# Attention over five start-up rounds: downsampled exponentials read straight from the scores' bank, and a new order of each engine's steps in a round

## The chip, the cores and the metric

The kernel runs on one core of one Trainium2 chip. The metric is the device time of one execution in microseconds (us); the kernel before took 924.17 us (median of three runs). All engines of the core run their own instruction streams and meet through semaphores: TensorE (PE; weight loads are shown apart as PEld), VectorE (DVE), ScalarE (ACT), GpSimd (POOL) and the queue SyncE (SP) that issues nearly all transfers.

## The reference, cut to what matters

For 4 batches of 8 heads, 576 positions and head size 64, attention is the sum of two branches, and its result goes through a gated layer and a squared-ReLU layer.

```
def sm_attn(qq, kk, vv):
    s = scale * np.matmul(qq, kk.transpose(0, 1, 3, 2))
    s = s - np.max(s, axis=-1, keepdims=True)
    a = np.exp(s)
    a = a / (np.sum(a, axis=-1, keepdims=True) + 1e-09)
    return np.matmul(a, vv)
q_d, k_d, v_d = ...          # means over groups of 4 positions: 144 positions
out_up = np.repeat(sm_attn(q_d, k_d, v_d), 4, axis=2)
mask = np.abs(pos[:, None] - pos[None, :]) < 4
...                          # out_local: softmax attention inside the mask
attn = out_up + out_local
x = silu(x @ w_gate) * (x @ w_val) @ w_out     # 2304 tokens, 512 -> 1536 -> 512
h = np.maximum(x @ w_in, 0.0)                  # 512 -> 2048 -> 512
return h * h @ w_out
```

## The kernel before, in words

Heads are taken in pairs: 4 pairs make a batch (`PAIRS`), 16 pairs make the whole input. Pairs 0 to 3 are computed in five **rounds** (n = 0 to 4) with little else to do for TensorE. From then on there are 48 **slots** in which the dense products of the first weight pass of one batch fill TensorE while the attention of the next pairs is spread between them, and then the chunks of the two layers with a seven-product scheme. The rounds occupy the first 47 us; the change is in them alone.

Each round n works on three pairs at once. What happens to one pair i, by names and lines:

- `pe_scores_loc` (L757) writes banded scores into the banks `sc`: two mask products (L763) and 40 small ones (L774). `dve_maximum_loc` (L1483) takes maxima (L1490) and writes scores minus maximum to `probs_l` (L1494), which frees `sc` for the next pair. `act_exp_loc` (L1166) takes exponentials in place; `dve_normalise_loc` (L1498) sums, adds, inverts, multiplies (L1503 to L1509), with its small sums kept in the last columns of bank `sd`. `pe_turn_loc1` and `pe_turn_loc2` transpose the result (L793, tile `tr`), ACT copies it out (L1178, L1182).
- `pe_scores_ds` (L779) writes the downsampled scores, three tiles of 144 columns, into bank `sd` (L788). `dve_maximum_ds` (L1512) takes maxima (L1515) and writes scores minus maximum to `probs_d` (L1519). `act_exp_ds` (L1169) takes exponentials of `probs_d` in place, one instruction of 432 columns (L1171). `dve_normalise_ds` (L1523) sums (L1527), adds, inverts, multiplies (L1534). `pe_turn_ds` transposes in two halves, each copied out by ACT (`act_move_ds`, L1189).
- `pe_values_loc` (L866) and `pe_values_ds` (L848) multiply by the values. ACT copies the downsampled part (`act_move_ods`, L1197), `dve_sum_branches` (L1545) adds the branches, `act_split_x` (L1206) and POOL's `split_x_lo` (L642) split the sum into a rounded part and a rest for the dense products.
- `pe_keep_busy` (L875) issues products whose result nobody reads: 8 in round 0 after the first scores, then 4, 4 and 5 in a middle round, 2 in the last.

**Feeding.** POOL makes the sums of four positions: `downsample_qk` (L613 to L623, for the next pair) and `downsample_v` (L631 to L636). The tile `v_grp` that the latter reads has one buffer: SP issues the load for the next pair (L384) only when `downsample_v` is done (`s_vds`), and everything behind it in SP's queue (weights L424, q and k L358, value windows L368 and L374) waits with it. POOL runs in its written order: in round 1 `downsample_qk(2)`, the rest of weight unit 0 (`first_weight_lo`, L675), `downsample_v(1)`; in round 2 `downsample_qk(3)`, `split_x_lo(0)`, `downsample_v(2)`; in round 3 `downsample_qk(4)`, `split_x_lo(1)`, `downsample_v(3)`, weight unit 1; then `split_x_lo(2)`. `first_weight_lo(i)` needs ACT's rounded copy of the weights (`act_weight`, L1275), which ACT makes for unit 0 in round 1, unit 1 in round 2 and unit 2 in round 3 (`ROUND_HI`), ahead of the first copy of transposed probabilities.

`pe_scores_ds(n)` opens round n on PE, ahead of `pe_scores_loc(n + 1)`. The first slot's dense product over pair 2 waits for the first half of `split_x_lo(2)` (`s_xlo`).

Of the kernel before, what the change touches and what calls it, by code (L numbers as in the profile page):

```python
# [165 lines left out]
def mlp_kernel(nc, qT, kT, v, w1_in, w1_out, w2_in, w2_out, out):  # L166
    ctx = ExitStack()
    with ctx:
        def sb(name, shape, dt=F32):
            return ctx.enter_context(nc.sbuf_tensor(name, shape, dt))  # L170
# [39 lines left out]
        ident = sb("ident", [P, P])  # L210
        max_l = sb("max_l", [P, 2, TJ])
        max_d = sb("max_d", [P, DT])
        credits = sb("credits", [P, 2])

        def late(name, shape, offset, dt=F32):
# [492 lines left out]
        def _(g):  # L708
# [26 lines left out]
            for ps in range(1, PASSES):  # L735
# [3 lines left out]
                for m in range(MT):  # L739
                    pool_out_lo(g, ps, m)  # L740

        def sums_loc(k):


            return sd[:, DT * DS + 2 * TJ * k:DT * DS + 2 * TJ * (k + 1)]
# [32 lines left out]

        def pe_scores_ds(pe, i):  # L779
            if i > 0:  # L780
                pe.wait_ge(s_subd, i)
                pe.wait_ge(s_norml, i)
            if i > PAIRS:
                pe.wait_ge(s_normd, i)
            pe.wait_ge(s_qkds, 3 * i + 3)
            for q in range(DT):
                for h in range(2):
                    last = nc.tensor.matmul(sd[64 * h:64 * h + 64, DS * q:DS * (q + 1)],  # L788
                                            q_ds[:, h, DQ * q:DQ * q + 64], k_ds[:, :], start=True, stop=True)
            last.then_inc(s_sd, 1)  # L790
# [81 lines left out]
        def pe_keep_busy(n):  # L872

            for _ in range(n):
                nc.tensor.matmul(mlp_ps[0][:, 0:LOC], ident16[:, :],  # L875
                                 mask[:, 0:TJ, :].rearrange("p j k -> p (j k)"), start=True, stop=True)

        def pe_round(pe, n):
            if n == 0:
                pe_scores_loc(pe, 0)  # L880
                pe_keep_busy(8)
            pe_scores_ds(pe, n)
            if n < PAIRS:
                pe_scores_loc(pe, n + 1)
            if n == PAIRS:
                pe_keep_busy(2)
                pe_first_in(pe, 0, 0, 0, 0, 0, KT - 2)
            if n > 0:
                pe_turn_ds(pe, n - 1, 0)
                if n < PAIRS:  # L890
                    pe_keep_busy(4)
                pe_turn_ds(pe, n - 1, 1)
                pe_values_loc(pe, n - 1)
                pe_values_ds(pe, n - 1)
            if n < PAIRS:
                pe_keep_busy(4)
                pe_turn_loc1(pe, n)
                pe_keep_busy(5)
                pe_turn_loc2(pe, n)

        def pe_slot(pe, g):
# [266 lines left out]

        def act_exp_ds(a, i):  # L1169
            a.wait_ge(s_subd, i + 1)  # L1170
            nc.scalar.activation(probs_d[:, :], probs_d[:, :], ACT.Exp, scale=SCALE / FACTOR ** 2)\  # L1171
              .then_inc(s_expd, 1)

        def act_move_loc1(a, i):
            a.wait_ge(s_turn1, i + 1)
# [33 lines left out]

        def act_round(a, n):  # L1210
            last = n == PAIRS
            if not last:
                act_exp_loc(a, n)
            for i in ROUND_HI.get(n, []):
                act_weight(a, i)
            if n > 0:
                act_move_ds(a, n - 1, 0)
            if n > 1:
                act_split_x(a, n - 2)
            if n > 0:  # L1220
                act_move_ds(a, n - 1, 1)
                if last:
                    act_exp_loc(a, n)
                act_move_ods(a, n - 1)
            if last:
                act_split_x(a, n - 1)
                act_exp_ds(a, n)
                return
            act_move_loc1(a, n)
            act_exp_ds(a, n)  # L1230
            act_move_loc2(a, n)

        def act_slot(a, g):

# [277 lines left out]
        def dve_maximum_ds(d, i):  # L1512
# [10 lines left out]
        def dve_normalise_ds(d, i):  # L1523
            total, den, inv = (sums_ds(i, k) for k in range(3))
            pd = probs_d[:, :].rearrange("p (q k) -> p q k", q=DT)
            d.wait_ge(s_expd, i + 1)
            nc.vector.tensor_reduce(total, pd, AX.X, ALU.add).then_inc(s_sumd, 1)  # L1527
            d.wait_ge(s_sumd, i + 1)
# [21 lines left out]

        def dve_round(d, n):
            last = n == PAIRS
            if not last:
                dve_maximum_loc(d, n)
            if n > 0:
                dve_normalise_ds(d, n - 1)
            if n > 1:
                dve_sum_branches(d, n - 2)
            if last:
                dve_maximum_loc(d, n)  # L1560
            if last:
                dve_sum_branches(d, n - 1)
                dve_maximum_ds(d, n)
                dve_normalise_loc(d, n)
            else:
                dve_normalise_loc(d, n)
                dve_maximum_ds(d, n)

        def dve_slot(d, g):
            for i in pairs_in(7, g):  # L1570
# [310 lines left out]
```

## Time and profile before

| | |
|---|---|
| median of 3 runs | 924.17 us (920.74 to 924.63) |
| the profiled execution | 926.48 us |
| its span in the trace | 924.7 us |
| outside the span | 1.8 us |
| TensorE busy | 909.2 us (98%) |
| VectorE, ScalarE, GpSimd busy | 650.9, 400.4, 219.8 us |
| granted TensorE clock, mean | 0.996 |

A row of the timeline has the start in us, the duration, the engine, the line and operation, the tile written and the tiles read with their shapes, how many instructions were merged, and in brackets the idle time of the engine ahead of it with what ended it. A tile name in a row is that of the program without buffer numbers; `mlp_ps` and `sd` are banks of PSUM. The profiled execution is 2.3 us longer than the median run.

### The profile page before, as it was taken

To read this page: it belongs to the slowest core of one execution; us is meant where nothing else is said; L and a number is where in the kernel's file an instruction comes from. 1 tells how busy PE (TensorE), PEld (TensorE's weight loads), DVE (VectorE), ACT (ScalarE), POOL (GpSimd) and SP (SyncE) were. 2 spreads that over 40 slices of the span, in tenths; PEclk is the share of its full clock that TensorE was granted. 3 is DMA by queue.
4 is the path that set the end of the run, shared out by engine and by line. 5 is a ranking of instruction groups with operands and counts; after the bars stand their busy time and mean duration, and the time that the engine had idled before them with its cause. 6 is when DMAs were issued, how large, how long until landed. Compare 5 with 4: busy or idle time off the path is not lost.

```text
span 924.7 us, 17274 instructions
## 1 busy us (share of the span) xinstructions
PE 909.2 (98%) x6762; PEld 879.0 (95%) x6762; DVE 650.9 (70%) x1112; ACT 400.4 (43%) x733; POOL 219.8 (24%) x278
## 2 busy tenths in 40 slices
PE   8899999999999999999999999999999999999998
PEld 5698999999999999999999999999999999999998
DVE  7685756564576757796757799585879575778775
ACT  3474555554446343455343445242535242525331
POOL 5784545452262000422000223000313000202000
PEclk9899999999999999999999999999999999999999
DMA  9953333231242020421311230010332020221422
GB/s 219 220 175 105 105 103 97 72 99 32 87 126 68 2 69 1 123 83 35 103 35 69 74 133 1 1 35 1 103 103 69 0 70 1 80 80 35 137 69 69
DMA packets 70881, 71.38 MB, mean 77 GB/s; under 512 B 27280, under 2 KB 58000, under 8 KB 70800
## 3 DMA queue, kind: packets, MB, share of 16 engines
q1 hardware_dynamic: 68496, 65.55, 24.3%
q10 hardware_dynamic: 2304, 4.72, 1.5%
q8 instruction: 54, 0.88, 0.4%
q14 instruction: 27, 0.22, 0.1%
HBM read 56.10 MB, written 14.16 MB: 76 GB/s over the span
## 4 chain that ended last, share of the span: by engine, by line
PE 85%; DVE 6%; ACT 3%; DMA 2%; issue 2%; POOL 1%; SPq 1%; ACTq 0%; DVEq 0%; POOLq 0%
PE mlp_ps L975 13%; PE mlp_ps L977 12%; PE mlp_ps L976 12%; PE sc L975 5%; PE sc L977 5%; PE sc L976 5%; PE xp L977 4%; PE xp L975 4%; PE xp L976 4%; PE sd L975 3%; PE sd L977 2%; PE sd L976 2%; PE tr L975 2%; PE tr L977 2%; PE tr L976 2%
## 5 line engine op out<-in xcount | busy, mean ns | idle before, releaser
L1388 ACT ACTIVATE wh_hi<-hbuf 128x384 fp32r<-128x384 f32 x144 | 70.8, 522 | 79.5 <-DVE hbuf L1674 57.1
L694 POOL TENSOR_TENSOR w_raw<-w_raw 128x256 f32<-128x256 f32 x16 | 14.3, 894 | 355.4 <-DMA w_raw<-w_in 355.4
L1682 DVE TENSOR_TENSOR wh_lo<-hbuf,wh_hi 128x384 fp32r<-128x384 f32 x144 | 76.5, 560 | 24.5 <-ACT wh_hi L1388 21.0
L1637 DVE TENSOR_TENSOR ring<-ring_raw,ring 128x768 fp32r<-128x768 f32 x96 | 90.9, 969 | 0.0
L1337 ACT ACTIVATE ring<-ring_raw 128x768 fp32r<-128x768 f32 x96 | 75.3, 836 | 28.8 <-DVE ring_raw L1631 28.5
L975 PE MATMUL mlp_ps<-ring,w_hi 128*128 128x384 f32 x240 | 80.3, 334 | 0.4 <-ACT snap L1368 0.4
L977 PE MATMUL mlp_ps<-ring,w_lo 128*128 128x384 f32 x240 | 80.2, 334 | 0.0
L976 PE MATMUL mlp_ps<-ring,w_hi 128*128 128x384 f32 x240 | 80.2, 334 | 0.0
L975 PE MATMUL mlp_ps<-wh_hi,w_hi 128*128 128x384 f32 x216 | 73.0, 338 | 2.3 <-DVE wh_lo L1682 1.2
L976 PE MATMUL mlp_ps<-wh_lo,w_hi 128*128 128x384 f32 x216 | 72.2, 334 | 0.0
L977 PE MATMUL mlp_ps<-wh_hi,w_lo 128*128 128x384 f32 x216 | 72.2, 334 | 0.0
L977 PE MATMUL sc<-wh_hi,w_lo 128*128 128x384 f32 x216 | 72.2, 334 | 0.0
L976 PE MATMUL sc<-wh_lo,w_hi 128*128 128x384 f32 x216 | 72.2, 334 | 0.0
L975 PE MATMUL sc<-wh_hi,w_hi 128*128 128x384 f32 x216 | 72.1, 334 | 0.0
L975 PE MATMUL mlp_ps<-xin,w_hi 128*128 128x288 f32 x216 | 65.9, 305 | 0.0
L976 PE MATMUL mlp_ps<-xin,w_hi 128*128 128x288 f32 x216 | 63.7, 295 | 0.0
L977 PE MATMUL mlp_ps<-xin,w_lo 128*128 128x288 f32 x216 | 63.5, 294 | 0.0
L704 POOL TENSOR_TENSOR w_lo<-w_raw,w_hi 128x512 fp32r<-128x512 f32 (+1 forms) x20 | 30.5, 1545 | 138.6 <-ACT w_hi L1311 138.6
L1674 DVE SCALAR_TENSOR_TENSOR hbuf<-hbuf 128x384 f32<-128x384 f32 x96 | 57.2, 629 | 1.4
L1362 ACT ACTIVATE hbuf<-sd 128x384 f32<-128x384 f32 x24 | 11.8, 492 | 99.3 <-PE sd L977 99.3
L975 PE MATMUL sd<-ring,w_hi 128*128 128x384 f32 x144 | 48.3, 335 | 0.6 <-ACT snap L1368 0.4
L976 PE MATMUL sd<-ring,w_hi 128*128 128x384 f32 x144 | 48.1, 334 | 0.0
(208 smaller groups left out, 2671.7 us busy)
## 6 DMA issues: line engine op xcount, KB each, us to landing
ring_raw<-x_whole SPq DMA_DIRECT2D x24, 384.0 KB, 3.7
ring_raw<-y_whole SPq DMA_DIRECT2D x24, 384.0 KB, 3.7
qk_sb<-qT SPq DMA_DIRECT2D x16, 288.0 KB, 3.3
qk_sb<-kT SPq DMA_DIRECT2D x16, 288.0 KB, 4.2
v_grp<-v SPq DMA_DIRECT2D x32, 144.0 KB
x_whole<-x_f ACTq DMA_DIRECT2D x16, 288.0 KB, 2.3
y_whole<-ypart SPq DMA_DIRECT2D x3, 1536.0 KB, 6.3
v_win<-v SPq DMA_DIRECT2D x64, 64.0 KB, 2.8
```

Of the source, the lines that this page charges most:

```text
L694: nc.gpsimd.tensor_tensor(block(5), block(7), block(4), ALU.add).then_inc(s_usum[i], 1)
L704: nc.gpsimd.tensor_tensor(w_lo[:, a:a + n], w_raw[:, a:a + n], w_hi[:, a:a + n].bitcast(F32), ALU.subtract).then_inc(s_olo[m], 1)
L975: nc.tensor.matmul(o, wh, xh, start=first, stop=False, skip_group_check=more)
L976: nc.tensor.matmul(o, wh, xl, start=False, stop=False, skip_group_check=more)
L977: return nc.tensor.matmul(o, wl, xh, start=False, stop=last, skip_group_check=more)
L1337: nc.scalar.activation(ring[:, SLOTS[g][p], 0, :, :], whole(g, p), ACT.Copy).then_inc(s_ophi, 1)
L1362: nc.scalar.activation(made_in(g, n, 0), BANK_1[n % 2], ACT.Copy).then_inc(s_snap1, 1)
L1388: nc.scalar.activation(hi[:, f, t, :], hbuf[:, e, :], ACT.Copy).then_inc(s_shhi, 1)
L1637: nc.vector.tensor_tensor(ring[:, SLOTS[g][p], 1, :, :], whole(g, p), ring[:, SLOTS[g][p], 0, :, :].bitcast(F32), ALU.subtract).then_inc(s ...
L1674: nc.vector.scalar_tensor_tensor(hbuf[:, e, :], hbuf[:, e, :], 0.0, hbuf[:, e, :], ALU.max, ALU.mult).then_inc(s_m, 1)
L1682: nc.vector.tensor_tensor(lo[:, f, t, :], hbuf[:, e, :], hi[:, f, t, :].bitcast(F32), ALU.subtract)\
```

## The change

For pairs 0 to 3 the subtraction of the maximum (L1519) and the separate row sum (L1527) go away. VectorE only scales the three maxima into a shift (`shift_d`), and ScalarE reads the scores from bank `sd` itself, in three instructions of 144 columns, each with its shift as bias and its row sum as second output (`total_d`). So bank `sd` stays taken until ScalarE is through: `pe_scores_ds` and `dve_normalise_loc`, whose sums lie in the same bank, wait for it. Round 4's pair (4) keeps the old form.

The order of each engine in a round is changed with it. PE: `pe_scores_ds(n + 1)` is issued at the end of round n between the two transposes of the local probabilities; `pe_scores_loc(n + 1)` stands between the two halves of `pe_turn_ds(n - 1)`; keep-busy products are 2 and 2 in a middle round. ACT: `act_move_ds(n - 1, 0)` leads, both exponentials follow, and `act_weight` goes to the very end of the round. VectorE: `dve_normalise_ds(n - 1)` leads, `dve_maximum_loc`, `dve_maximum_ds`, `dve_sum_branches(n - 2)` and `dve_normalise_loc` follow. POOL's and SP's own orders are untouched.

```diff
         def pe_scores_ds(pe, i):
             if i > 0:
-                pe.wait_ge(s_subd, i)
+                if i <= PAIRS:
+                    pe.wait_ge(s_expd, exps_ds(i))
+                else:
+                    pe.wait_ge(s_subd, i)
                 pe.wait_ge(s_norml, i)
...
         def pe_round(pe, n):
+            last = n == PAIRS
             if n == 0:
                 pe_scores_loc(pe, 0)
                 pe_keep_busy(8)
-            pe_scores_ds(pe, n)
-            if n < PAIRS:
-                pe_scores_loc(pe, n + 1)
-            if n == PAIRS:
+                pe_scores_ds(pe, 0)
+            if n > 0:
                 pe_keep_busy(2)
+            if last:
                 pe_first_in(pe, 0, 0, 0, 0, 0, KT - 2)
             if n > 0:
                 pe_turn_ds(pe, n - 1, 0)
-                if n < PAIRS:
-                    pe_keep_busy(4)
+            if not last:
+                pe_scores_loc(pe, n + 1)
+            if n > 0:
                 pe_turn_ds(pe, n - 1, 1)
                 pe_values_loc(pe, n - 1)
                 pe_values_ds(pe, n - 1)
-            if n < PAIRS:
-                pe_keep_busy(4)
+            if not last:
+                pe_keep_busy(2)
                 pe_turn_loc1(pe, n)
-                pe_keep_busy(5)
+                pe_scores_ds(pe, n + 1)
                 pe_turn_loc2(pe, n)
...
         def act_exp_ds(a, i):
             a.wait_ge(s_subd, i + 1)
-            nc.scalar.activation(probs_d[:, :], probs_d[:, :], ACT.Exp, scale=SCALE / FACTOR ** 2)\
-              .then_inc(s_expd, 1)
...
+            if i > 0:
+                a.wait_ge(s_turnd, 2 * i)
+                a.wait_ge(s_dend, i)
+            for q in range(DT):
+                cols = slice(DS * q, DS * (q + 1))
+                nc.scalar.activation(probs_d[:, cols], sd[:, cols], ACT.Exp, bias=shift_d[:, q:q + 1],
+                                     scale=SCALE / FACTOR ** 2, accum_out=total_d[:, q:q + 1]).then_inc(s_expd, 1)
...
         def act_round(a, n):
             last = n == PAIRS
+            if n > 0:
+                act_move_ds(a, n - 1, 0)
             if not last:
                 act_exp_loc(a, n)
-            for i in ROUND_HI.get(n, []):
-                act_weight(a, i)
+                act_exp_ds(a, n)
             if n > 0:
-                act_move_ds(a, n - 1, 0)
+                act_move_ds(a, n - 1, 1)
             if n > 1:
                 act_split_x(a, n - 2)
...
             act_move_loc1(a, n)
-            act_exp_ds(a, n)
             act_move_loc2(a, n)
+            for i in ROUND_HI.get(n, []):
+                act_weight(a, i)
...
         def dve_normalise_loc(d, i):
             d.wait_ge(s_expl, i + 1)
             d.wait_ge(s_sd, i + 1)
+            if i < PAIRS:
+
+                d.wait_ge(s_expd, exps_ds(i + 1))
...
         def dve_maximum_ds(d, i):
-            if i > 0:
-                d.wait_ge(s_turnd, 2 * i)
+            if i < PAIRS:
+                if i > 0:
+                    d.wait_ge(s_expd, exps_ds(i))
+                nc.vector.tensor_scalar(shift_d[:, :], max_d[:, :], -SCALE / FACTOR ** 2, 0.0, ALU.mult, ALU.add)\
+                  .then_inc(s_subd, 1)
+                return
...
         def dve_normalise_ds(d, i):
+            d.wait_ge(s_expd, exps_ds(i + 1))
+            if i < PAIRS:
+                total = total_d[:, :]
+            else:
+                nc.vector.tensor_reduce(total, pd, AX.X, ALU.add).then_inc(s_sumd, 1)
```

`exps_ds(n)` counts the exponentials of the first n pairs: three for each of pairs 0 to 3, one from pair 4 on.

## Rows read from the trace of the kernel before

**Rows 1.** The page: busy time by engine, and the transfers' share in 40 slices.
```profile
PE 909.2 (98%) x6762; PEld 879.0 (95%) x6762; DVE 650.9 (70%) x1112; ACT 400.4 (43%) x733; POOL 219.8 (24%) x278
...
DMA  9953333231242020421311230010332020221422
```

**Rows 2.** Busy time of each engine in the stretch behind the rounds.
```profile
43.46:100.00 56.54, 55.91 (x700) 50.82 (x699) 41.70 (x80) 33.52 (x66) 37.28 (x51) 1.00 0.47 135
```

**Rows 3.** The chain that ended last, 0 to 64 us: start, us, what.
```profile
25.89 8.51 DMA ypart<-w_in
...
46.78 0.64 PE xp L848 x8
```

**Rows 4.** Timeline of ACT in the rounds.
```profile
13.13 0.55 ACT L1171 ACTIVATE probs_d<-probs_d 128x432 f32<-128x432 f32 x1
...
16.14 1.06 ACT L1275 ACTIVATE w_hi<-ypart 128x1024 fp32r<-128x1024 f32 x1 [0.73 <-DMA ypart<-w_in]
...
25.57 0.39 ACT L1189 ACTIVATE probsT_d<-tr 72x288 f32<-72x288 f32 x1
...
28.01 0.29 ACT L1197 ACTIVATE o_ds<-xp 128x144 f32<-128x144 f32 x1 [1.03 <-PE xp L848]
...
34.43 1.06 ACT L1275 ACTIVATE w_hi<-ypart 128x1024 fp32r<-128x1024 f32 x1 [3.47 <-DMA ypart<-w_in]
```

**Rows 5.** Timeline of PE in the rounds.
```profile
8.67 0.96 PE L788 MATMUL sd<-k_ds,q_ds 128*64 128x144 f32 x12
...
22.74 1.34 PE L774 MATMUL sc<-qk_sb 64*58 64x64 f32 x40
...
26.02 0.52 PE L793 MATMUL tr<-ident,probs_d 128*72 128x128 f32 x3 [0.94 <-ACT probsT_d L1189]
...
35.83 0.85 PE L793 MATMUL tr<-ident,probs_d 128*72 128x128 f32 x3 [2.29 <-ACT probsT_d L1189]
```

**Rows 6.** Two 1 us stretches; last: granted clock, DMA share, GB/s.
```profile
35.00:36.00 1.00, 0.17 (x1) 0.17 (x2) 0.11 (x1) 1.00 (x3) 0.99 (x2) 0.82 0.86 203
...
42.00:43.00 1.00, 1.00 (x11) 0.66 (x11) 0.70 (x2) 0.51 (x2) 0.86 (x2) 0.77 0.79 128
```

**Rows 7.** Timeline of DVE, rounds 2 and 3.
```profile
23.98 0.82 DVE L1503 TENSOR_REDUCE sd<-probs_l 128x10 f32<-128x640 f32 x1
...
25.30 0.82 DVE L1509 TENSOR_TENSOR probs_l<-probs_l,sd 128x640 f32<-128x640 f32 x1
...
26.68 0.61 DVE L1519 TENSOR_TENSOR probs_d<-sd,max_d 128x432 f32<-128x432 f32 x1
...
28.05 0.82 DVE L1494 TENSOR_TENSOR probs_l<-sc,max_l 128x640 f32<-128x640 f32 x1
...
30.12 0.61 DVE L1527 TENSOR_REDUCE mlp_ps<-probs_d 128x3 f32<-128x432 f32 x1 [1.25 <-ACT probs_d L1171]
30.77 0.17 DVE L1530 TENSOR_SCALAR mlp_ps<-mlp_ps 128x3 f32<-128x3 f32 x1
...
32.45 0.82 DVE L1503 TENSOR_REDUCE sd<-probs_l 128x10 f32<-128x640 f32 x1
```

**Rows 8.** Timeline of POOL in the rounds.
```profile
22.75 0.73 POOL L631 TENSOR_TENSOR v_tmp<-v_grp 72x256 f32<-72x256 f32 x1 [3.11 <-DMA v_grp<-v]
...
27.53 0.48 POOL L623 TENSOR_TENSOR k_ds<-qk_tmp 128x144 f32<-128x144 f32 x1
...
40.84 0.72 POOL L631 TENSOR_TENSOR v_tmp<-v_grp 72x256 f32<-72x256 f32 x1 [1.72 <-DMA v_grp<-v]
...
43.08 2.36 POOL L675 TENSOR_TENSOR w_lo<-ypart,w_hi 128x1024 fp32r<-128x1024 f32 x1
45.88 1.55 POOL L642 TENSOR_TENSOR xin<-x_f,xin 128x288 fp32r<-128x288 f32 x2 [0.44 <-ACT xin L1206]
```

**Rows 9.** Timeline of the queue SP: issues of the `v_grp` loads.
```profile
25.05 0.79 SPq L384 DMA_DIRECT2D v_grp<-v  x2
...
34.69 0.77 SPq L384 DMA_DIRECT2D v_grp<-v  x2
```

More of the change, by code:

```diff
@@ L212, in mlp_kernel @@
         max_d = sb("max_d", [P, DT])
+        shift_d = sb("shift_d", [P, DT])
+        total_d = sb("total_d", [P, DT])
         credits = sb("credits", [P, 2])
@@ L740, in _, with exps_ds @@
                     pool_out_lo(g, ps, m)
+        def exps_ds(n):
+            return DT * min(n, PAIRS) + max(n - PAIRS, 0)
         def sums_loc(k):
@@ L1170, in act_exp_ds @@
             a.wait_ge(s_subd, i + 1)
-            nc.scalar.activation(probs_d[:, :], probs_d[:, :], ACT.Exp, scale=SCALE / FACTOR ** 2)\
-              .then_inc(s_expd, 1)
+            if i >= PAIRS:
+                nc.scalar.activation(probs_d[:, :], probs_d[:, :], ACT.Exp, scale=SCALE / FACTOR ** 2)\
+                  .then_inc(s_expd, 1)
+                return
[6 more added lines that the diff above has]
+                                     scale=SCALE / FACTOR ** 2, accum_out=total_d[:, q:q + 1]).then_inc(s_expd, 1)
         def act_move_loc1(a, i):
@@ L1211, in act_round @@
             last = n == PAIRS
+            if n > 0:
+                act_move_ds(a, n - 1, 0)
             if not last:
                 act_exp_loc(a, n)
-            for i in ROUND_HI.get(n, []):
-                act_weight(a, i)
+                act_exp_ds(a, n)
             if n > 0:
-                act_move_ds(a, n - 1, 0)
+                act_move_ds(a, n - 1, 1)
             if n > 1:
                 act_split_x(a, n - 2)
+            if last:
+                act_exp_loc(a, n)
             if n > 0:
-                act_move_ds(a, n - 1, 1)
-                if last:
-                    act_exp_loc(a, n)
                 act_move_ods(a, n - 1)
@@ L1516, in dve_maximum_ds @@
             d.wait_ge(s_maxd, i + 1)
-            if i > 0:
-                d.wait_ge(s_turnd, 2 * i)
+            if i < PAIRS:
[3 more added lines that the diff above has]
+                  .then_inc(s_subd, 1)
+                return
+            d.wait_ge(s_turnd, 2 * i)
             nc.vector.tensor_tensor(probs_d[:, :].rearrange("p (q k) -> p q k", q=DT), tiles,
@@ L1525, in dve_normalise_ds @@
             pd = probs_d[:, :].rearrange("p (q k) -> p q k", q=DT)
-            d.wait_ge(s_expd, i + 1)
-            nc.vector.tensor_reduce(total, pd, AX.X, ALU.add).then_inc(s_sumd, 1)
-            d.wait_ge(s_sumd, i + 1)
+            d.wait_ge(s_expd, exps_ds(i + 1))
[3 more added lines that the diff above has]
+                nc.vector.tensor_reduce(total, pd, AX.X, ALU.add).then_inc(s_sumd, 1)
+                d.wait_ge(s_sumd, i - PAIRS + 1)
             nc.vector.tensor_scalar(den, total, EPS, float(FACTOR), ALU.add, ALU.mult).then_inc(s_dend, 1)
@@ L1552, in dve_round @@
             last = n == PAIRS
-            if not last:
-                dve_maximum_loc(d, n)
             if n > 0:
                 dve_normalise_ds(d, n - 1)
-            if n > 1:
+            if last:
                 dve_sum_branches(d, n - 2)
-            if last:
                 dve_maximum_loc(d, n)
-            if last:
                 dve_sum_branches(d, n - 1)
                 dve_maximum_ds(d, n)
-                dve_normalise_loc(d, n)
             else:
-                dve_normalise_loc(d, n)
+                dve_maximum_loc(d, n)
                 dve_maximum_ds(d, n)
+                if n > 1:
+                    dve_sum_branches(d, n - 2)
+            dve_normalise_loc(d, n)
         def dve_slot(d, g):
```

## The prediction

> **What bounds the kernel now.** I read the page first: TensorE is busy 98% of the span [rows 1]. Then the busy time by stretch: behind the rounds it is busy 55.91 of 56.54 us [rows 2], so from about 47 us on the work is rigid, and the change can only move the moment at which that dense work begins. The chain of waits for the first 64 us came third. It shows that the rounds are not bound by one engine. A weight load of 8.51 us sits in the chain, and the last step of the rounds, the downsampled values of pair 3, starts at 46.78 and ends at 47.42 [rows 3]. That 47.42 is the mark I move below; the dense product over pair 2 follows it directly.
>
> The timelines say why. On ScalarE the rounded copy of weight unit 2 waits 3.47 us for its load, and everything behind it on ScalarE waits too [rows 4]. TensorE then stands 2.29 us before the second half of a transpose, where the round before had 0.94 [rows 5], and in this gap the granted clock falls: 0.82 on average in the microsecond from 35, 0.77 in that from 42, with 0.5 between, so slow from about 35.64 to 42.46 [rows 6]. Those are 6.8 us at 1.2 instead of 2.4 GHz; the same transposes took 0.85 us instead of 0.52 [rows 5]. At that ratio of 1.63 the slow stretch cost 6.8 x (1 - 1/1.63) = 2.6 us. Beside this a second chain runs, through transfers and POOL: the value load for `downsample_v` is what POOL waits for, 3.11 us before 22.75 and 1.72 us before 40.84 [rows 8], and the transfer engines are at nine tenths or more in the first two slices of 23 us each [rows 1].
>
> **The change on VectorE and ScalarE.** VectorE loses the subtraction (0.61) and the sum (0.61) and gains a shift like the 0.17 us scaling: 1.05 us a round less [rows 7]. A round of VectorE ran 32.45 - 23.98 = 8.47 us, 1.25 of it idle before the sum [rows 7]; its own work was thus 7.2 and becomes about 6.2. ScalarE loses one exponential of 0.55 us and gains three of 144 columns. The nearest row, a copy of 128x144 out of PSUM, is 0.29 [rows 4]. No row shows an accumulator output or a bias per partition. From below the three cost no less than the one they replace, 0.55; from above I let each need a second instruction of the same 0.29, 1.74 in all. I take 1.1, near three times 0.29 with a little for the sums.
>
> The Trainium skill, page "ScalarE: Activation LUTs", section "What ACT_TABLE_LOAD costs", gives 280 ns + 0.833 ns a column for an exponential with a pointer bias and an overlap of 93 ns. An estimate by that page is three times 0.40 less two overlaps, 1.0 us, without a price for the sum. That speaks against splitting one instruction into three; the sum of this text does not use it.
>
> **One middle round, new order.** I count from N, the end of the local normalisation on VectorE. TensorE: first transposes and downsampled scores, about 0.6 and 0.9; copy and last transpose and copy, to N + 2.0; fillers and first transpose half, to 2.6. VectorE meanwhile has finished `dve_normalise_ds` (sum gone, 0.95) and `dve_maximum_loc` (twice 0.82 [rows 7]), at 2.6 too. Local scores of the next pair, 0.3 + 1.34 [rows 5], to 4.3; second transpose half (0.52), to 4.8. Only then may ScalarE write `probs_d`: exponentials to 5.9. Only then may VectorE touch the bank: local normalisation, from the row 23.98 to the end of the row 25.30 2.14 us [rows 7], to 8.1. So the new round is 8.1 us long. The added wait costs what it hides: behind the waiting normalisation nothing is queued on VectorE but the next round, and TensorE waits for it after its last two fillers. VectorE's 1.05 us is gone into that wait: the round is bound by a chain TensorE - ScalarE - VectorE, not by VectorE. Against the undisturbed round of 8.47 this is 0.4 shorter, against its busy part longer.
>
> **Start.** Round 0: the downsampled scores are in at 8.67 + 0.96 = 9.63 [rows 5], maximum 0.6, shift 0.2, exponentials 1.1, normalisation 2.15 and some 0.2 of signals: N0 = 13.9 (before, that normalisation went ahead of the downsampled maxima). N1 = 22.0, N2 = 30.1 by the period.
>
> **The moved weight copies.** `act_weight` now stands last. What goes: ScalarE's 3.47 us stall, with the 1.35 us it added to TensorE's gap and the 2.6 of the slow clock. What comes: unit 0 is copied at N1 + 2.0 = 24.0 to 25.1 instead of 16.14 [rows 4]. POOL's rest of unit 0 (2.37 [rows 8]) then runs to 27.5, `downsample_v(1)` (43.08 - 40.84 = 2.25 [rows 8]) to 29.7, `downsample_qk(3)` (28.01 - 22.75 - 2.25 = 3.0 [rows 8]) to 32.7. Before, the latter ended at 27.53 + 0.48 = 28.0; 3.1 of the 7.9 us were covered by POOL's wait, the rest is not. TensorE wants these sums for the scores of pair 3 at N2 + 0.6 = 30.7: 2.0 late, the only delay of the main chain. N3 = 30.1 + 8.1 + 2.0 = 40.2. The copies of units 1 and 2 wait for nothing by then: unit 2's load landed at 34.4 [rows 3], also when issued 4 us later it is there at 42.
>
> From N3: transposes, scores of pair 4, last transpose 1.8, fillers and the first dense products 1.1, two transpose halves with their copies (0.5 and 0.39 each [rows 4, 5]) 1.8: TensorE could do the values of pair 3 at 44.9 and be done at 45.6, 1.8 before the mark.
>
> **The other chain.** POOL on: `split_x_lo(0)` 1.55 [rows 8] to 34.2, `downsample_v(2)` to 36.5, `downsample_qk(4)` to 39.5 (TensorE wants it at 40.8, fine), `split_x_lo(1)` to 41.0, then `downsample_v(3)`. Its load landed at 40.84 before, issued at 34.69 [rows 8, 9]. Now it is issued behind `downsample_v(2)` and SP's other issues, about 36.8. SP is also held from 25.05 [rows 9] to 29.7 by the load before that one. I take the landing as unchanged, since the transfer engines have work queued for that long: a load issued at 25.89 landed 8.5 us later [rows 3]. So `downsample_v(3)` ends at 43.3, unit 1 (2.36 [rows 8]) at 45.7, the first half of `split_x_lo(2)` at 46.5. Before, it ended at 45.88 + 0.8 = 46.7 and was covered by TensorE's values to 47.42. Now it is what TensorE's first product over pair 2 waits for. The mark moves from 47.42 to 46.5: a gain of 0.9 us. The main chain's other 0.9 is lost behind POOL. So dropping 3.47 us of stall and 2.6 us of slow clock brings one: the value load, POOL's fixed order and the later weight unit take the rest.
>
> **Sum.** 926.48 - 0.9 = 925.6 us for a profiled execution; the median stands 2.3 lower, 924.17 - 0.9 = 923.3 us.
>
> **Rivals.**
>
> First, the clock falls in the rounds: slower. After its two fillers of round 0 TensorE waits from 11.5 to 13.9, 2.4 us, as long as the 2.29 us gap in which it fell before [rows 5, 6]; and a middle round keeps 4 of 13 fillers. TensorE's work on the round's chain is 0.6 + 0.9 + 0.3 + 0.5 + 1.6 + 0.5 = 4.4 us; at 1.63 a slow round is 2.8 longer. Three of them, 8.4, put the main chain's end at 45.6 + 8.4 = 54.0, 7.5 behind the forecast's mark: 923.3 + 7.5 = 930.8 us. Two give 51.2, 928.0 us, 3.8 over 924.17; so it counts as slower from the third slow round on. For it: gap and fillers. Against: the other gaps of the new round are 0.9 and 1.0 us, and a gap of 0.94 left the clock alone [rows 5].
>
> Second, the transfers run dry while SP is held to 29.7. Then the load for pair 3 takes its old 6.15 us from its issue, 36.8 + 6.15 = 43.0, and all behind it is 1.2 to 2 us later: 924.5 to 925.5 us. For it: 4.7 us of no issues. Against: the queue of 8.5 us.
>
> Third, the loads land earlier, because the x stores (ScalarE's queue) go later and SP's later windows no longer compete; the mark is then the main chain's 45.6 or, with cheap exponentials (0.55: 0.55 less in each of four rounds), 43.4. That is 922.4 to 920.2. More than 4.6 us of gain needs the value load of pair 3 some 4 us before 40.84, with transfer engines already full: hardly.
>
> **How the numbers follow.** Forecast 0.53, transfers dry 0.18, earlier loads 0.14, clock 0.15 (of which 0.10 for at least three slow rounds or their like, 0.05 for one or two). Dear exponentials (1.74) add 0.64 a round, up to 2 us at the mark, inside the range. The range 920.3 to 928.0 leaves out the worst of the clock case and a sliver below. Taking 0.5% (4.6 us) as what a measurement can tell from no change: faster 0.06 (part of the third rival and what I can't see), slower 0.12, same 0.82.
>
> **What would show it.** Right: no idle of ScalarE before L1275 from a load; rounds of about 8 us between local normalisations; VectorE idle some 1.5 us before each L1503 with ScalarE as releaser; POOL's unit 0 ending near 27.5 and scores of pair 3 waiting for POOL; values of pair 3 near 45; the first dense product over pair 2 released by POOL near 46.5; clock 1.0 throughout. Wrong: a clock of 0.5 after 13.9 (first rival), transfer share well under 0.9 between 28 and 32 us (second), three exponentials far from 1.1 us, or a mark outside 44 to 49 us.

## The result, and the profile after

| | before | after |
|---|---|---|
| median | 920.70 us (920.02 to 924.63, 6 runs) | 930.99 us (929.54 to 932.38, 6 runs) |
| ratio | | 1.0097, interval 1.0079 to 1.0115 |
| profiled execution, span | 926.5, 924.7 us | 932.4, 930.6 us |
| first dense product over pair 2 ("the mark") | 47.35 us | 51.76 us |
| slow clock in the first 60 us | 6.8 us | 13.6 us |

The change costs about 1%, well clear of the noise; the forecast was no change that can be measured. The table holds the first surprise as well: the profiled execution of before was 6 us longer than the median of its runs. The second profile of the same kernel, further down, explains it.

The page of after, its engines and transfers. Beside [rows 1] the transfers' share of the second slice fell from 9 to 6.

```profile
PE 907.3 (98%) x6728; PEld 877.8 (94%) x6728; DVE 647.8 (70%) x1108; ACT 403.1 (43%) x753; POOL 219.6 (24%) x278
...
DMA  8663324221241010331211140010332020221422
```

The chain that ended last, after, first 56 us (start, us, what). Where before had a weight load, now 8.81 us without any work of the chain precede POOL's rest of weight unit 0; then POOL, a value load of 6.98 us and POOL again lead to the dense product.

```profile
18.66 8.81 issue
27.51 2.36 POOL w_lo L677
...
39.29 6.98 DMA v_grp<-v
...
50.95 0.76 POOL xin L644
51.76 0.40 PE mlp_ps L986
```

The timelines of after: ScalarE's copy of unit 0, POOL, SP's issue of the second value load (before: 25.05, [rows 9]), VectorE's local normalisation and TensorE. What the reader is to see: copy at 26.39 instead of 16.14 [rows 4], POOL 8.85 us idle for it, the value load of pair 2 out at 32.13 and that of pair 3 at 38.82, VectorE 3.86 us idle for the exponentials, TensorE 1.68 us idle for POOL at the mark.

```profile
26.39 1.05 ACT L1297 ACTIVATE w_hi<-ypart 128x1024 fp32r<-128x1024 f32 x1
...
27.51 2.36 POOL L677 TENSOR_TENSOR w_lo<-ypart,w_hi 128x1024 fp32r<-128x1024 f32 x1 [8.85 <-ACT w_hi L1297]
...
46.34 0.74 POOL L633 TENSOR_TENSOR v_tmp<-v_grp 72x256 f32<-72x256 f32 x1 [1.95 <-DMA v_grp<-v]
...
32.13 0.77 SPq L386 DMA_DIRECT2D v_grp<-v  x2
...
38.82 0.86 SPq L386 DMA_DIRECT2D v_grp<-v  x2
...
22.16 0.83 DVE L1528 TENSOR_REDUCE sd<-probs_l 128x10 f32<-128x640 f32 x1 [3.86 <-ACT probs_d L1192]
...
14.71 0.72 PE L803 MATMUL tr<-ident,probs_l 128*128 128x128 f32 x4 [2.77 <-DVE probs_l L1534]
...
51.76 0.40 PE L986 MATMUL mlp_ps<-xin,w_hi 128*128 128x288 f32 x1 [1.68 <-POOL xin L644]
```

Stretches of 1 us of after (the last three columns: granted clock, transfers' share, GB/s). The clock falls at about 15.2 and is back at 18.6, is slow again from 32.2 to 39.1 and from 52.7 to 56.1; the transfers stand at 0.12 at 22 us and at nothing at 28.

```profile
15.00:16.00 1.00, 1.00 (x10) 0.76 (x10) 1.00 (x2) 0.52 (x1) 0.13 (x1) 0.59 0.91 135
...
22.00:23.00 1.00, 0.63 (x8) 0.44 (x8) 0.83 (x1) 0.32 (x2) 0.00 (x0) 1.00 0.12 29
...
28.00:29.00 1.00, 1.00 (x27) 0.79 (x23) 0.30 (x1) 0.35 (x1) 1.00 (x1) 1.00 0.00 0
...
32.00:33.00 1.00, 0.80 (x8) 0.80 (x8) 0.96 (x3) 0.00 (x0) 1.00 (x3) 0.62 0.00 0
```

The new exponentials, ScalarE, after: three pairs of an exponential and a read of the sum, 20.83 to 22.03, 1.2 us.

```profile
20.83 0.38 ACT L1192 ACTIVATE probs_d<-sd,shift_d 128x144 f32<-128x144 f32 x1 [1.02 <-issue]
21.11 0.19 ACT L1192 ACTIVATION_READ_ACCUMULATOR probs_d<-sd,shift_d 128x1 f32 x1
...
21.82 0.21 ACT L1192 ACTIVATION_READ_ACCUMULATOR probs_d<-sd,shift_d 128x1 f32 x1
```

### The profile page after: what moved, and what is told of

It reads as the page before. It is cut to its first block, busy times and chain, and to the rows that moved or that the text cites. A ratio compares the mean times of both kernels' runs of the same rounds, so it can differ in the third digit from the quotient of the medians.

```text
span 930.6 us, 17225 instructions
## 1 busy us (share of the span) xinstructions
PE 907.3 (98%) x6728; PEld 877.8 (94%) x6728; DVE 647.8 (70%) x1108; ACT 403.1 (43%) x753; POOL 219.6 (24%) x278
## 4 chain that ended last, share of the span: by engine, by line
PE 83%; DVE 6%; ACT 3%; issue 3%; POOL 3%; DMA 1%; SPq 0%; DVEq 0%; ACTq 0%; POOLq 0%
PE mlp_ps L986 12%; PE mlp_ps L988 12%; PE mlp_ps L987 12%; PE sc L986 5%; PE sc L987 5%; PE sc L988 5%; PE xp L987 4%; PE xp L986 4%; PE xp L988 4%; PE sd L986 2%; PE sd L987 2%; PE sd L988 2%; PE sc L780 2%; PE tr L986 2%; PE tr L988 2%
## 5 line engine op out<-in xcount | busy, mean ns | idle before, releaser
L986 PE MATMUL sd<-ring,w_hi 128*128 128x384 f32 x144 | 48.3, 335 | 0.6 <-ACT snap L1390 0.4
L986 PE MATMUL xp<-wh_hi,w_hi 128*128 128x384 f32 x144 | 48.1, 334 | 0.0
```

The source lines that it names most:

```text
L986: nc.tensor.matmul(o, wh, xh, start=first, stop=False, skip_group_check=more)
```

## The experiments

Three theories stood at the start; the expectations also call them theory 1, 2 and 3. **Feed**: the late copy of weight unit 0 holds POOL, POOL holds the value loads, and these hold SP's whole queue. **Clock**: longer gaps and fewer products of `pe_keep_busy` let the clock fall. **Round**: the new round is longer by itself. Behind a mark come about 879 us (before 926.5 - 47.35 = 879.1, r_before 920.4 - 41.4 = 879.0), and up to 882 us in the executions that also wait or run at the slow clock behind it.

### Single repairs of the changed kernel

**e1**: ScalarE's copies back near their old place.

```diff
                 act_exp_loc(a, n)
+                for i in ROUND_HI.get(n, []):
+                    act_weight(a, i)
                 act_exp_ds(a, n)
...
             act_move_loc2(a, n)
-            for i in ROUND_HI.get(n, []):
-                act_weight(a, i)
```

> The changed kernel with one thing undone: ScalarE's weight copies stand behind the local exponential (near their old place) and not at the end of the round. In the changed kernel unit 0 was copied at 26.39, POOL began its rest at 27.51 after 8.85 us of idle time, the next value load left at 32.13 and the first dense product over pair 2 came at 51.76. Theory 1 (feed: the late copy holds POOL, POOL holds the value loads and with them all transfers): copy near 20, in the gap before the exponentials, POOL's unit 0 done near 22.5, second value load leaves near 25.5, transfers no longer run dry from 22 to 33 us, dense product at 46 to 48; time 4 to 6 us under the changed kernel's, about 925 to 927. Theory 2 (clock: fewer fillers and longer gaps): dense product moves by under 1 us, time 930 to 931, slow stretches stay. Theory 3 (the round's own chain of TensorE, ScalarE, VectorE is the limit): local normalisations keep their distance of 8.4 to 11.7 us and the time stays within 1 us.

Measured 928.76 us, 1.0088 of before (1.0071 to 1.0105), mark 48.45, second value load at 26.71. POOL's wait for unit 0 shrank from 8.85 us to 2.20:

```profile
20.24 2.35 POOL L677 TENSOR_TENSOR w_lo<-ypart,w_hi 128x1024 fp32r<-128x1024 f32 x1 [2.20 <-ACT w_hi L1297]
```

The feed is mended, the mark moved by 3.3 us, the median by 2.2: half of what the feed theory expected. The transfers still ran low (0.07 to 0.24 in four of the five stretches of 1 us from 22 to 27 us): SP waited 7.4 us in all, from 14 to 50 us, for TensorE's products of the values ahead of its value windows. The clock was slow for 6.8 us.

**e3**: the changed kernel with fillers in TensorE's waits.

```diff
                 pe_values_loc(pe, n - 1)
+                if not last:
+                    pe_keep_busy(6)
                 pe_values_ds(pe, n - 1)
             if not last:
-                pe_keep_busy(2)
+                pe_keep_busy(8 if n else 18)
```

> The changed kernel with more products whose result nobody reads, put into TensorE's waits: 18 instead of 2 at the end of round 0, 6 added before the downsampled values and 8 instead of 2 before the local transposes of middle rounds. Theory 2 (clock): the granted clock stays at 1.0 up to 30 us at least, slow time falls from 13.4 us to under 7, time 3 us or more under the changed kernel's. Theory 1 (feed): round 1 is 1.6 us shorter (no slow clock from 15.4 to 18.7), and as the weight copy follows round 1 the whole feed moves by that much; 929 to 930, with POOL's long wait for the copy of unit 0 still 7 us or more.

Measured 926.32 us, 1.0063 (1.0048 to 1.0078), mark 47.54, clock 1.0 throughout. POOL still waited 8.39 us:

```profile
25.84 2.37 POOL L677 TENSOR_TENSOR w_lo<-ypart,w_hi 128x1024 fp32r<-128x1024 f32 x1 [8.39 <-ACT w_hi L1299]
```

So 4.7 us of the loss hang on the clock: 1.7 us because all of the feed starts earlier, the rest in the slow stretches at 32 and 53 us. Here both theories gave a number and the clock theory's was right.

**e4**: POOL's rest of unit 0 moved to round 2, behind `downsample_v(2)`.

```diff
-                if n == 1:
-                    first_weight_lo(g, nc.gpsimd, 0)
                 downsample_v(g, n)
+                if n == 2:
+                    first_weight_lo(g, nc.gpsimd, 0)
```

> The changed kernel with POOL's rest of weight unit 0 moved from round 1 (ahead of the second downsampling of values) to round 2 (behind the third); ScalarE's order stays as changed. Theory 1 (feed): same gain as putting ScalarE's copy back: second value load leaves near 25 and not at 32, transfers busy from 22 to 33 us, dense product at 46 to 48, time 925 to 927. Theory 2 and 3: within 1 us of the changed kernel.

Measured 928.80 us, 1.0086 (1.0066 to 1.0107), mark 49.27. The second value load left at 25.45, as expected, but ScalarE's copy of unit 1 and the third downsampling then stood in POOL's way at 35.5, and the clock was slow in three stretches, 10.3 us in all. Feed from the other side: 2.2 us again, half of what was expected; the four runs spread from 926.65 to 930.50, and the profiled one is the slowest of them.

**e7**: e1 and e3 together.

> The changed kernel with ScalarE's weight copies behind the local exponential and with the fillers (18, 6, 8); POOL's order as in both kernels. The two single repairs brought the first dense product over pair 2 from 51.76 to 48.45 and 47.54. If feed and clock are the two losses and add up: clock 1.0, dense product at 45 to 46.5, time 924 to 925.5, still 3.5 to 5 us over before, the rest being the round itself (local normalisations 8.4 us apart against 7.5 in the undisturbed execution of before). If the round costs nothing: 920 to 922.

Measured 925.17 us, 1.0031 of before (1.0012 to 1.0049), mark 45.23. Within the numbers expected: the two losses overlap and make 5.8 us together. What remains over before is 3.9 us by the medians (925.17 against 921.29 on this chip) and 2.9 by the ratio. It lies in the round itself: with a clock of 1.0 and no wait of TensorE for POOL, local sums are 28.73 - 20.36 = 8.37 us apart, and VectorE waits for the exponentials in each round.

```profile
20.36 0.83 DVE L1530 TENSOR_REDUCE sd<-probs_l 128x10 f32<-128x640 f32 x1 [2.98 <-ACT probs_d L1194]
...
28.73 0.83 DVE L1530 TENSOR_REDUCE sd<-probs_l 128x10 f32<-128x640 f32 x1 [2.23 <-ACT probs_d L1194]
```

### What the kernel before really does

**r_before**: the kernel before, unchanged, profiled again.

> The kernel before, unchanged, profiled once more: the profiled execution of before took 926.5 us and its median over more runs is 920.5, so the sum may have been anchored on an execution with a disturbance of its own. Theory 2 (clock): this execution takes 920 to 922 us, its clock stays at 1.0 through the rounds, ScalarE's wait for weight unit 2 is under 2.5 us, and the first dense product over pair 2 comes at 42 to 44 us and not at 47.35. Theory 1 alone: 924 to 926 us and the mark at 47 us again.

Measured 921.84 us median (920.34 to 924.55), its profiled execution 920.37 us with the mark at 41.41 and a clock of 1.0. The rows answer those of [rows 4], [rows 7], [rows 8] and [rows 3]: ScalarE waits 0.48 us and not 3.47 for the load of unit 2; local sums are 31.19 - 23.71 = 7.48 us apart and not 8.47; POOL has the value load of pair 3 at 35.99 and not 40.84; the values of pair 3 are at 40.33.

```profile
30.19 1.06 ACT L1275 ACTIVATE w_hi<-ypart 128x1024 fp32r<-128x1024 f32 x1 [0.48 <-DMA ypart<-w_in]
...
23.71 0.82 DVE L1503 TENSOR_REDUCE sd<-probs_l 128x10 f32<-128x640 f32 x1
...
31.19 0.82 DVE L1503 TENSOR_REDUCE sd<-probs_l 128x10 f32<-128x640 f32 x1
...
35.99 0.73 POOL L631 TENSOR_TENSOR v_tmp<-v_grp 72x256 f32<-72x256 f32 x1 [1.84 <-DMA v_grp<-v]
...
40.33 0.71 PE L848 MATMUL xp<-probsT_d,v_ds 72*64 72x144 f32 x8
41.41 0.40 PE L975 MATMUL mlp_ps<-xin,w_hi 128*128 128x288 f32 x1 [0.38 <-POOL xin L642]
```

The same program runs with its loads landing 4 to 5 us earlier or later: unit 2 of the weights at 30.2 or 34.4, the values of pair 3 at 36.0 or 40.8. Why is not shown; it begins with the value load of pair 1, issued at 15.04 here and landed by 18.7, issued at 14.45 in the other and landed at 22.7. The forecast was built on an execution with late loads: its stall of 3.47 us, its slow clock and its mark at 47.4 are absent from this one. By the times this one is the usual one: of 94 runs of before next to the experiments and in the result, 11 took more than 924 us. In it TensorE waits 0.38 us for POOL at the mark, so that is all that a faster chain of POOL's alone could gain, and a faster TensorE alone would gain nothing.

### Parts of the change, one at a time, on the kernel before

**e2**: only the copies go to the end of the round.

```diff
-            for i in ROUND_HI.get(n, []):
-                act_weight(a, i)
             if n > 0:
                 act_move_ds(a, n - 1, 0)
...
             act_move_loc2(a, n)
+            for i in ROUND_HI.get(n, []):
+                act_weight(a, i)
```

> The kernel before with one thing of the change: ScalarE's weight copies go to the end of the round. Theory 1 (feed): unit 0 is copied near 22 instead of 16.1, POOL's unit 0 runs 23 to 25.4, the downsampled values of pair 1 come 2.5 us later, the value load of pair 2 too; against that ScalarE's stalls of 2.1 and 3.5 us on weight loads go. Net -1 to +3 us against before. Theory 3: no harm at all, a gain of 2 to 4 us, since what made the change slow is the round's new order and not the copies.

Measured 926.34 us, 1.0056 (1.0041 to 1.0071), mark 46.17. This edit alone costs more than half of the whole loss. POOL waited 6.33 us for unit 0, TensorE then 2.31 us for POOL at the mark, and after this gap the clock was slow from 47.6 to 51.0, which goes with 880.5 us behind the mark where 879 are usual. Both theories were too kind (5.9 us lost, where the first had at most 3): the gain that they counted, from ScalarE's stalls, belongs to the execution with late loads.

```profile
23.64 2.37 POOL L675 TENSOR_TENSOR w_lo<-ypart,w_hi 128x1024 fp32r<-128x1024 f32 x1 [6.33 <-ACT w_hi L1275]
...
46.17 0.40 PE L975 MATMUL mlp_ps<-xin,w_hi 128*128 128x288 f32 x1 [2.31 <-POOL xin L642]
```

**e10**: unit 0 stays, only units 1 and 2 go to the end (`if n in (2, 3): act_weight(a, n - 1)`).

> The kernel before with ScalarE's copies of weight units 1 and 2 at the end of rounds 2 and 3, unit 0 left where it was. Moving all three cost 5 us. Theory feed: POOL needs unit 0 ahead of a value load, unit 1 only later, so this costs nothing: 919.5 to 921.5, the upper end of the runs lower than before's (no stall of 3.5 us when a weight load is late). If late copies cost as such: 923 or more.

Measured 920.79 us, 0.9992 (0.9977 to 1.0008), 920.00 to 922.63 over 12 runs where before on the same chip had 919.64 to 927.27 over 35. With e2 this puts the harm on unit 0, the one that a value load stands behind. As the feed theory expected, moving the other two costs nothing. That it also trims the upper end fits the missing wait, but 12 runs don't prove it.

**e8**: only the new exponentials, old order. The edit is the diff of `act_exp_ds`, `dve_maximum_ds`, `dve_normalise_ds` and `pe_scores_ds` above, without the added wait of `dve_normalise_loc`.

> One part alone: the new exponentials (read from the scores' bank, with shift and row sums, no subtraction, no separate sum) in the order of the kernel before; the wait of the local normalisation for them is not needed in that order and left out. Theory 1: feeding is untouched, so within 2 us of before, 919 to 922; VectorE does 1 us less a round and the downsampled scores of the next pair start up to 0.7 us later. Theory 3 (the exponentials' longer chain ScalarE to TensorE is what costs): 923 or more.

Measured 923.04 us, 1.0019 (1.0006 to 1.0032), mark 44.03. The time is at the edge of theory 3's numbers (923 or more), and the trace decides for the longer chain: TensorE waits for the exponentials ahead of the next downsampled scores in every round, where before waited for nothing, and VectorE's saved 1 us turns up as idle time.

```profile
22.54 0.96 PE L797 MATMUL sd<-k_ds,q_ds 128*64 128x144 f32 x12 [0.76 <-ACT probs_d L1190]
```

**e12**: as e8, but ScalarE issues the exponentials ahead of `act_move_ods`.

```diff
+                if not last:
+                    act_exp_ds(a, n)
                 act_move_ods(a, n - 1)
...
             act_move_loc1(a, n)
-            act_exp_ds(a, n)
+            if n == 0:
+                act_exp_ds(a, n)
```

> New exponentials in the old order, but from round 1 on issued on ScalarE ahead of the copy of the downsampled values (where ScalarE stood idle 1.04 and 0.72 us) and not behind that of the local transposes. Theory bank (the scores' bank is released too late): TensorE's waits of 0.76 us vanish from round 1 on, downsampled scores 7.5 us apart and not 8.3, first dense product over pair 2 at 41.5 to 42.5, time 920.5 to 921.5. Theory length (three reads with sums are 1.2 us against 0.55, and ScalarE has no room): 922.5 to 924.

Measured 922.05 us, 1.0007 (0.9996 to 1.0019), mark 43.51. From round 1 on the wait is gone. In rounds 2 and 3 the scores are 7.48 us apart, as in before. Round 1 took 8.47: VectorE's scaling of the maxima into the shift, 0.17 us elsewhere, took 2.47 there, ScalarE's exponentials started late for it, and TensorE stood 0.99 us before the last transpose. Why it can take so long is told at the end.

```profile
15.29 0.96 PE L797 MATMUL sd<-k_ds,q_ds 128*64 128x144 f32 x12 [0.76 <-ACT probs_d L1190]
...
19.08 2.47 DVE L1542 TENSOR_SCALAR shift_d<-max_d 128x3 f32<-128x3 f32 x1
...
23.50 0.33 PE L802 MATMUL tr<-ident,probs_l 128*128 128x128 f32 x1 [0.99 <-ACT probsT_l L1197]
23.76 0.96 PE L797 MATMUL sd<-k_ds,q_ds 128*64 128x144 f32 x12
...
31.24 0.96 PE L797 MATMUL sd<-k_ds,q_ds 128*64 128x144 f32 x12
```

So the trace puts the cost of e8 on the moment at which the scores' bank is released, not on the length of the exponentials: where the bank is free in time, the three longer instructions cost the round nothing. The times say it less firmly. 922.05 us lies between the two theories' numbers, and the intervals of e8 and e12 overlap. The mark came out 1 us later than expected, all of it in the first rounds: round 0's downsampled scores ended 1.0 us later than in r_before, and round 1 lost another 1 us as told.

**e13**: e12 with maxima in PSUM and the copies of e10.

> As e12, with the maxima in the scores' bank and ScalarE's copies of weight units 1 and 2 at the end of rounds 2 and 3. Theory bank: level with before, 920 to 921.5, and not faster, since TensorE was busy without a gap in the undisturbed rounds of before (7.5 us with 13 products nobody reads) and POOL's first half of the split of pair 2 ended 0.1 us before the dense product: VectorE's 1 us a round has nobody waiting for it. If VectorE had been the bound of those rounds: 917 to 919.

Measured 923.06 us, 1.0021 (1.0003 to 1.0039), 920.17 to 926.30, in two clusters, at 920 to 922 and at 924 to 926. The median lies above every number expected of the bank theory; the lower cluster lies close to them (920.17 to 921.77). The rounds are as expected: downsampled scores 7.5 us apart in all of them, with a scaling of 0.16 us each time. The profiled execution is of the upper cluster, and its feed was late: the value load of pair 3 came 3.10 us after POOL wanted it, TensorE stood 1.54 us at the mark until 43.77, and the clock was slow from 43.3 to 50.1. Not shown: how the lower cluster looks inside, and why five of ten runs took more than 924 us here, where 11 of 94 of before did. Nothing here beats before.

**e9**: only the new order of PE, ScalarE and VectorE, with the old exponentials (the diff of `pe_round`, `act_round`, `dve_round`).

> The other part alone: the new order of all engines with the old subtraction, exponential and row sum. Theory feed: unit 0 of the weights is copied at 24 to 26 us, POOL waits 6 us or more for it, the second value load leaves after 30 us, and the time is 927 to 930. The wait of the local normalisation for the bank is gone, but the subtraction waits for the transposes of the pair before, so rounds are shorter by only 0.5 to 1 us. If instead the exponentials made most of the change's loss: 921 to 924.

Measured 927.15 us, 1.0055 (1.0038 to 1.0073), mark 46.94: as the feed theory said, with the copy at 23.16 and the second value load at 28.90, each about 1 us earlier than it expected. POOL waited 8.01 us:

```profile
24.29 2.35 POOL L675 TENSOR_TENSOR w_lo<-ypart,w_hi 128x1024 fp32r<-128x1024 f32 x1 [8.01 <-ACT w_hi L1277]
```

e2, with the late copies alone, had 1.0056. So where the feed bounds both, the rest of the new order costs nothing that these runs can tell. The loss beyond the copies needs the new exponentials in the new order.

**e5** and **e6**: both of POOL's weight rests moved off the value chain, once on e2 and once on e7.

```diff
-                if n == 1:
+                downsample_v(g, n)
+                if n == 2:
                     first_weight_lo(g, nc.gpsimd, 0)
-                downsample_v(g, n)
-                if n == PAIRS - 1:
-                    first_weight_lo(g, nc.gpsimd, 1)
...
                 split_x_lo(g, n - 1)
+                first_weight_lo(g, nc.gpsimd, 1)
```

> The kernel before with ScalarE's weight copies at the end of the round and POOL's rests of weight units moved off the value chain: unit 0 behind the third downsampling of values, unit 1 behind both splits of the last round. Theory 1 (feed): the second value load leaves near 25 us as before, neither ScalarE nor POOL waits for weights ahead of attention steps; 5 us or more under the version that moved only the copies (926.3), so 918 to 921. Theory 3 (order of the round): within 1 us of 926.3.

> The changed kernel with both repairs and the fillers: weight copies behind the local exponential, POOL's units 0 and 1 off the value chain, 18, 6 and 8 products whose result nobody reads. Theory 1 with 2 (feed and clock together are the whole loss): clock 1.0, second value load leaves near 24, transfers busy throughout, dense product over pair 2 at 43 to 45.5 us, time 919 to 922, level with before. Theory 3 (the new chain of the round costs on its own): 923 to 926, with local normalisations 8.4 us apart although nothing feeds late.

Measured 923.71 us, 1.0035 (1.0019 to 1.0051), and 928.31 us, 1.0069 (1.0042 to 1.0097), with marks at 44.45 and 46.17. Both lie outside the numbers of every theory. e5 gained 2.6 us over e2, which speaks for the feed; e6 lost 3 us against e7. Inside the rounds of e5, unit 0's rest, now at 32.73, held POOL ahead of the sums for pair 4: TensorE stood 2.29 us for them, and the clock was slow from 38.0 to 41.4. Behind the mark come 882 us instead of 879 in both: unit 1's rest was now too late for the dense products themselves, and TensorE waited behind the mark for it (1.1 and 0.9 us) and for the downsampled sums queued behind it on POOL (1.5 us each). The repair moved the wait, it did not remove it; of the orders tried, POOL's written order of both kernels is the better one.

**e11**: e8 with the maxima kept in the scores' bank.

```diff
-            nc.vector.tensor_reduce(max_d[:, :], tiles, AX.X, ALU.max).then_inc(s_maxd, 1)
+            top = max_d[:, :] if i >= PAIRS else sd[:, DT * DS + 6 * TJ:DT * DS + 6 * TJ + DT]
+            nc.vector.tensor_reduce(top, tiles, AX.X, ALU.max).then_inc(s_maxd, 1)
```

> New exponentials in the old order, with the three maxima kept in the scores' bank, so that VectorE's scaling into the shift reads PSUM and not SBUF. With maxima in SBUF that scaling took 0.17 us or 0.53, 1.09 and 2.77 us, and the long ones ended when a running instruction of POOL ended. If POOL and VectorE exclude each other on SBUF in that form of instruction: every scaling under 0.25 us; time 0 to 1.5 us under the 923.0 of its twin. If the long ones are waits for something else: still 0.5 us and more in some rounds. TensorE's wait of 0.76 us a round for the exponentials ahead of the next scores stays.

Measured 923.25 us, 1.0015 (0.9997 to 1.0034): no time won, but the question is answered, below.

## Why the prediction was wrong

**The anchor failed first.** "That 47.42 is the mark I move below" took one profiled execution as the kernel. The warning stood in the same table: runs of 920.7, 924.2 and 924.6 beside a profile of 926.5. The 924.17 that the sum starts from is itself 3.5 us over the median of six runs. In the usual execution the mark is at 41.4 and the round at 7.48 us (r_before). Against that, my own walk, with the new mark at 46.5, would have said 5.1 us slower, not 0.9 faster. The stall of 3.47 us, the 1.35 us of gap and the 2.6 us of slow clock, all counted as gains, are not there to be gained: e2 removed the stall and lost 5.9 us.

**"I take the landing as unchanged, since the transfer engines have work queued for that long"** failed second. No row had shown such a load either: out at about 36.8 and landed at 40.84 is 4.0 us, where the same load took 6.15 before [rows 8, 9]. The queue was seen in the execution with late loads; after ran dry, 0.12 to 0.42 from 22 to 28 us and nothing from 28 to 30. The load of pair 3 landed at 46.34, not 40.84. This is the second rival; its mechanism was right and its price of 1.2 to 2 us was wrong, since it kept the issue at 36.8 and the load at 6.15 us, and they became 38.82 and 7.5. The mark stands 51.76 - 46.5 = 5.3 us behind the forecast's, and this landing alone is 5.5 us late: from it to the mark are 5.4 us, where the walk had 5.7. Terms ahead of it were short as well: the value load of pair 2 left at 32.13 (29.7 in my walk) and that of pair 3 at 38.82 (36.8).

**Why those were short.** N0 was 14.66 and not 13.9 (the downsampled scores were in 0.3 us later, the scaling took 0.53 and not 0.2). N1 was 24.32 and not 22.0: on top of N0's 0.8 the clock fell in the 2.77 us gap that I had put at 2.4 and had named as the first rival. I gave it 0.15, against a row of mine in which a gap of 2.29 us had brought it down, and let it count as slower only from the third slow round on. It came in three stretches, 13.6 us in all, and e3 prices it at 4.7 us. Against it I had set that a gap of 0.94 left the clock alone; what stood beside the 2.77 us was the nearer row, 2.29. The 930.8 us of that rival is near the measured 930.99, by luck of the sum: clock and feed shared it.

**What held.** The exponentials: 1.21 us for 1.1 forecast. The round bound by the chain TensorE - ScalarE - VectorE: local sums 8.37 us apart in e7 and in the first two rounds of e3, both at full clock, 8.1 forecast. The wait of `dve_normalise_loc` for ScalarE is there in each round, but 2.2 to 3.9 us where I had 1.5. POOL's unit 0 as what holds the loads, TensorE waiting for POOL ahead of the scores of pair 3 (0.28 us and not 2.0, since TensorE came late itself), and POOL as what releases the mark. VectorE's saved microsecond bringing nothing: also right, though for a reason that I had only half, since in r_before TensorE fills the rounds almost without a gap (one of 0.20 us from 8 to 38 us).

**The account.** From 920.7 to 931.0: the new exponentials with the old order are 1.7 to 2.3 us (e8), by the traces through the late release of the bank (e12). The new order with them, feed and clock repaired, makes 2.9 to 3.9 (e7). The feed and the clock, overlapping, make 5.8 (e7 against after); alone, 2.2 (e1) and 4.7 (e3). From the other side, the late copies alone lose 5.9 (e2), the rest of the new order adds nothing that can be told from it (e9), and the new exponentials add 3.8 to e9, with 13.6 us of slow clock where e9 has 3.4. That points to what the two make together, the wait of VectorE for the bank above all. But no run has the new exponentials in the new order without this wait, so what part of the 1 to 2 us between e8 and e7 it is, and what part the new order of TensorE is, stays open.

## What to carry to other kernels

Before a gain is counted on a stall, look whether the stall is there in the median execution: here a profile 0.6% over the median showed another path than the usual runs take. A step off the critical path that is moved late must be followed through every in-order queue behind it; here one copy on ScalarE held POOL, POOL a single load buffer, and that buffer the whole transfer queue. And when an engine reads a bank directly to spare a copy, count until when it holds the bank.

## What the runs showed of the hardware

Two things I had not expected. The scaling of three maxima (128x3, SBUF to SBUF, VectorE) takes 0.17 us, or until an instruction of POOL's ends: 0.53 us at 10.61 in after, 1.50 in e4, 1.09 and 2.77 us in e8, 2.47 in e12. The 2.77 us one of e8, VectorE and then POOL, from their timelines (start, duration, engine):

```profile
26.89 2.77 DVE L1539 TENSOR_SCALAR shift_d<-max_d 128x3 f32<-128x3 f32 x1
...
26.71 1.54 POOL L644 TENSOR_TENSOR xin<-x_f,xin 128x288 fp32r<-128x288 f32 x2
28.22 0.72 POOL L633 TENSOR_TENSOR v_tmp<-v_grp 72x256 f32<-72x256 f32 x1
28.91 0.72 POOL L634 TENSOR_TENSOR v_tmp<-v_grp 72x256 f32<-72x256 f32 x1
29.77 0.72 POOL L638 TENSOR_TENSOR v_ds<-v_tmp 72x256 f32<-72x256 f32 x1
```

It ends at 29.66, in POOL's pause between 29.63 and 29.77, after three rows that follow each other without one. With the maxima read from PSUM all four took 0.16 us in e11, and all four in e13:

```profile
27.01 0.16 DVE L1540 TENSOR_SCALAR shift_d<-sd 128x3 f32<-128x3 f32 x1
```

The page "SBUF — State Buffer" of the Trainium skill, section "Who interferes with whom", has the reason: such an operation of VectorE, with source and destination in SBUF, can take a pair of ports that it shares with POOL, and whoever comes second waits for the whole instruction of the other. The trace agrees, and with PSUM as the source the wait is gone; VectorE's normalisation of 128x640, with one operand in SBUF and one in PSUM, keeps its 0.82 us beside POOL, as the page has it too. But the row above waited for more than one instruction: for all that stood on POOL without a pause. So did the 2.47 us one of e12. Those of 0.53 us in after and 1.50 in e4 ended with one instruction of POOL's although the next followed at once; what decides is not shown. The wait mattered once: in e12 it lay on the chain that TensorE waited for, and round 1 took 8.47 us where e13, the same order with the maxima in PSUM, took 7.49. In e8 it cost TensorE 0.09 us (a wait of 0.85 instead of 0.76), and the times of e8 and e11 are level.

And an exponential with a row sum is two instructions on ScalarE, 0.38 and 0.19 us, that overlap to 0.36 us a pair: three such pairs in 1.21 us. The forecast's 1.1 us stood on three copies of 0.29 with a little for the sums. The estimate that it quotes from the Trainium skill (page "ScalarE: Activation LUTs", section "What ACT_TABLE_LOAD costs"), 0.40 us for an exponential and 1.0 for three, fits the instruction, and what it leaves out, as it says, are the sums.
